# Two chained top-1 expert layers: the second layer's router scores taken from the first layer's output matmuls

## Chip, cores and metric

One Trainium2 chip, one core of it. Times are microseconds (us) of device time for one launch; lower is better. The engines are TensorE (PE: matmuls, and PEld: its weight loads), VectorE (DVE), ScalarE (ACT), GpSimd (POOL) and SyncE (SP); SP, ACT and POOL also issue DMAs, each in the order of its own program.

## What is computed

The reference has three stages over 14,336 tokens of 192 features: a causal 7-tap convolution along the sequence, a layer of experts with a skip rule and a residual, and a second layer of experts. Cut to what matters:

```python
x = conv(x, softmax(weight))                     # 4 x 3584 tokens, D = 192
# layer 1 (m = 0): E = 8 experts, F = 1024
do_compute = x @ w_skip > 0
e = argmax(x @ w_gate);  gate = softmax(x @ w_gate)[e]
x1 = x + (gate * (relu(x @ w1[e]) @ w2[e]) if do_compute else 0)
# layer 2 (m = 1): its own experts, a second gate
e = argmax(x1 @ w_gate2); gate = softmax(x1 @ w_gate2)[e]
out = gate * sigmoid(x1 @ w_output_gate2)[e] * (relu(x1 @ w1'[e]) @ w2'[e])
```

## The kernel before

All five engines run programs written out by hand; order on an engine is program order, and semaphores alone order the engines among each other. There is no scheduler.

**The front** (`Fori(0, B)` by `GPB` = 4, so 16 groups of 896 tokens) convolves, transposes the rows, computes the 25 router scores of each token (`scoreT`: skip, gate 1, gate 2, output gate 2), picks the bucket of each token, and scatters the rows of 196 floats into DRAM with 7 indirect DMAs per group from POOL (L432). Tokens that layer 1 computes go to buckets 0 to 7, skipped ones directly to a bucket of layer 2 (8 to 15).

**The expert stages** (`m` = 0, then 1) walk tiles of 256 tokens, expert by expert: 33 tiles for m = 0, 60 for m = 1. A tile g on PE: the hidden matmuls of four pairs c (L1086, L1095), then for each of 8 chunks j the output matmuls into banks 4 and 6 (L1110 with the high part `hh`, 384 columns, since high and low half of `w2` lie side by side; L1117 with the low part `hl`, 192 columns). ACT turns each pair into `hh` (L607), DVE into `hl` (L815, `h_low`). The rows of the tile with their gate come by a DMA that ACT issues between pairs 1 and 2 into the one buffer `xkeep` (L612). DVE's `result` multiplies the banks by the gate and adds x (L885, L891).

**Routing inside m = 0.** The rows that tile g-1 produced are routed to layer 2 while tile g is computed. PE transposes `y_rows` (L1045, L1046), ACT copies the transposes out (L565, L566), PE multiplies them with the second layer's gates (L1056, L1057, fp32). On DVE `choose` finds the expert (L831 to L845), `gate` its weight (L851 to L857), and `places` the row in the bucket (L864 to L872), for which PE counts ranks (L1063, L1065) after chunk j = 5. POOL's `send` does this in order: wait until the DMAs of the previous send have landed (`sent`), copy `y_rows` into `s_rows` (L447) and signal `copied`, take a quarter of the next expert's `w2` (L419), wait for `slots` from `places`, and issue two indirect DMAs (L453). In DVE's program of tile g the order is: `h_low` 0, `flags`, `h_low` 1 and 2, a piece of the next expert's w1 (L686), `h_low` 3, `x_turn` (L802, L803), `choose`, `x_low` (L808, L809), `gate`, `places`, `result`.

The waits that matter, before:

```python
# POOL, send(r)
pool.wait_ge(s["sent"], r * 32 + 16)
nc.gpsimd.tensor_copy(s_rows[:], y_rows[:]).then_inc(s["copied"], 1)
# ACT, tile g, between pairs 1 and 2
act.wait_ge(s["yrows_ready"], g + 1)
act.dma_start(xkeep[:], tile_rows(g, off)).then_inc(s["keep_in"], 16)
```

Of the kernel before, what the change touches and what calls it, by code (L numbers as in the profile page):

```python
# [24 lines left out]
FAR = 1.0e6  # L25
# [5 lines left out]
def program(nc, x, weight_rev, w_skip, gate1, gate2, out_gate2, w1_all, w2_all, out):  # L31
# [5 lines left out]
    HD = D // H  # L37
# [13 lines left out]
    ROW = D + 4  # L51
    GATE, TOK = D, D + 1
# [13 lines left out]
    with ctx:  # L66
# [3 lines left out]
        def sem(name):  # L70
# [11 lines left out]
        routerB = sb("routerB", [128, QUAD])  # L82
        rank_down = sb("rank_down", [128, E])
# [11 lines left out]
        xwin = sb("xwin", [W, GPB, WPG, D])  # L95
# [4 lines left out]
        scoreT = sb("scoreT", [128, 2, W])  # L100
        tok_int = sb("tok_int", [128, GPB * WPG], I32)
# [37 lines left out]
        w2 = sb("w2", [128, 2, FC, 2, D], F32R)  # L139
# [7 lines left out]
        y_part = sb("y_part", [128, SUB, D])  # L147
        s_rows = sb("s_rows", [128, SUB, ROW])
        yT = sb("yT", [128, 2, T])
        out_i = sb("out_i", [128, SUB], I32)  # L150

        SC = bank[7][:, 0:2 * W].rearrange("p (h i) -> p h i", i=W)

# [3 lines left out]
        consts_in, consts_pool, kern_in, kern_step, kern_out, toep_in, kern_e = map(sem, (  # L157
            "consts_in", "consts_pool", "kern_in", "kern_step", "kern_out", "toep_in", "kern_e"))
# [3 lines left out]
        win_in = [sem(f"win_in{q}") for q in range(GPB)]  # L162
# [3 lines left out]
            "scoreT_ready", "scoreT_copied", "scores_ready", "z_ready", "e_ready", "hot_ready", "rank_ready"))  # L166
        slots_ready, route_step, ones_ready, counted, table_step, tables_ready, first_filled, filled = map(sem, (
# [7 lines left out]
                 "y_ready", "yrows_ready", "yT_ready", "yT_copied", "scores", "z",  # L175
# [51 lines left out]

        def load_weights(eng, expert, par, f=slice(0, F), c=slice(0, FC), count=16 * PIECES):
# [41 lines left out]

        def settle(eng):


            eng.sem_inc(settled, 1)
# [7 lines left out]
        def _(sp):  # L282
            sp.dma_start(kern[:], weight_rev).then_inc(kern_in, 16)

            def load_windows(b, q):

                at = (b * S + q * WPG * W) * D
                sp.dma_start(xwin[:, q, :, :], bass.AP(windows.tensor, at, [[D, W], [W * D, WPG], [1, D]])
                             ).then_inc(win_in[q], 16)
                first = 1 if q == 0 else 0  # L290
                for k in range(4):
                    sp.dma_start(xhalo[k * QUAD:k * QUAD + HALO, q, first:, :],
                                 bass.AP(windows.tensor, at + (first * W - HALO) * D + k * HD2,
                                         [[D, HALO], [W * D, WPG - first], [1, HD2]])).then_inc(win_in[q], 16)
# [5 lines left out]
            sp.dma_start(toep[:], bass.AP(rev_w.tensor, 0, [[1, W], [TAPS_PAD, H], [1, W]])  # L300
                         ).then_inc(toep_in, 16)

            for q in range(1, GPB):
                load_windows(0, q)
# [91 lines left out]
        def _(pool):  # L396
# [39 lines left out]
            for m in range(2):  # L436
# [27 lines left out]
                with pool.Fori(0, E // 2) as half:  # L464
                    for par in range(2):
                        e = half * 2 + par
                        first, end = tiles.of(e)
                        def piece(i):
                            low2(e + (m * E + 1), 1 - par, i)
# [687 lines left out]
```

## Time and profile before

| | |
|---|---|
| median of 3 runs | 1124.97 us (1124.86 to 1124.97) |
| the profiled execution | 1125.92 us, span 1124.0 us |
| PE busy | 1052.6 us, 94% |
| DVE busy | 705.7 us, 63% |
| ACT busy | 528.2 us, 47% |
| POOL busy | 383.2 us, 34% |
| chain that ended last | PE 83%, issue 6%, POOL 4% |

The span is what the trace covers; the 1.9 us beyond it lie outside. Busy shares are means over three stages with different limits, so the argument goes by stage: the front ends near 183 us with POOL's last scatter, m = 0 runs from there to about 558 us, m = 1 to the end. A busy share of PE counts overlapping matmuls, so distances between starts are used for what a matmul costs.

### The profile page before, as it was taken

How to read it: one execution, taken by the hardware profiler on the slowest of the kernel's cores; microseconds unless marked ns; L12 is line 12 of the kernel's file. 1: busy time of each engine (PE TensorE's matmuls, PEld its weight loads, DVE VectorE, ACT ScalarE, POOL GpSimd, SP SyncE). 2: the span in 40 equal slices, each digit the busy share in tenths (PEclk: the TensorE clock that was granted, in tenths of full speed). 3: DMA queues.
4: the chain of work that ended last, by engine and by line, in shares of the span. 5: the costliest groups of instructions: out<-in, count | busy, mean ns of one | idle time of the engine just before them, and what ended most of it. 6: DMA issues, size and time to landing. Idle time of an engine off the chain costs nothing.

```text
span 1124.0 us, 32029 instructions
## 1 busy us (share of the span) xinstructions
PE 1052.6 (94%) x8478; PEld 991.9 (88%) x8479; DVE 705.7 (63%) x2264; ACT 528.2 (47%) x1190; POOL 383.2 (34%) x420
## 2 busy tenths in 40 slices
PE   6888756999999999999699999999999999999997
PEld 6666645999999999999699999999999999999997
DVE  0555663787888888888745565555555556565554
ACT  1545531444444444545345455554545455454443
POOL 2577774233323333333313232222323223223212
PEclk8998986999999999999889999999999999999999
DMA  8654424433434344434253343433434334223332
GB/s 235 196 155 155 129 83 138 116 87 84 87 80 96 85 99 100 90 82 107 58 141 95 74 110 66 111 81 80 114 78 114 64 93 96 63 59 69 63 64 49
DMA packets 252850, 110.90 MB, mean 99 GB/s; under 512 B 170499, under 2 KB 247798, under 8 KB 252832
## 3 DMA queue, kind: packets, MB, share of 16 engines
q1 hardware_dynamic: 210856, 62.45, 26.3%
q0 software_dynamic: 14560, 27.96, 7.1%
q10 hardware_dynamic: 27416, 20.30, 6.6%
q14 instruction: 13, 0.11, 0.0%
q8 instruction: 5, 0.08, 0.0%
HBM read 79.48 MB, written 33.08 MB: 100 GB/s over the span
## 4 chain that ended last, share of the span: by engine, by line
PE 83%; issue 6%; POOL 4%; DVE 2%; DMA 2%; ACT 1%; ACTq 1%; POOLq 0%; SPq 0%; DVEq 0%
PE bank L1095 32%; PE bank L1110 26%; PE bank L1117 12%; PE bank L1086 5%; POOL buckets L432 4%; PE bank L1057 2%; PE bank L1056 1%; PE bank L955 1%; DMA buckets<-rows,slot_i 1%; PE bank L1045 1%; PE bank L1046 1%; ACT rows L519 1%; PE bank L1018 1%; PE bank L1019 0%; DMA toep_halo<-rev_w 0%
## 5 line engine op out<-in xcount | busy, mean ns | idle before, releaser
L1110 PE MATMUL bank<-w,hh 128*128 128x384 f32 x1488 | 444.3, 361 | 1.0 <-DVE hl L815 1.0
L1117 PE MATMUL bank<-w,hl 128*128 128x192 f32 x1488 | 363.8, 255 | 0.0
L815 DVE SCALAR_TENSOR_TENSOR hl<-bank,hh 128x512 fp32r<-128x512 f32 x372 | 252.6, 689 | 127.4 <-ACT hh L607 124.5
L607 ACT ACTIVATE hh<-bank 128x512 fp32r<-128x512 f32 x372 | 221.4, 598 | 161.5 <-PE bank L1095 155.5
L1117 PEld LDWEIGHTS bank<-w,hl 128*128 128x128 f32 x1488 | 282.8, 191 | 0.0
L1110 PEld LDWEIGHTS bank<-w,hh 128*128 128x128 f32 x1488 | 280.2, 188 | 2.1 <-DVE hl L815 1.2
L458 POOL DMA_INDIRECT out<-y_rows,out_i x120 | 117.3, 978 | 413.9 <-DVE out_i L893 382.6
L1095 PE MATMUL bank<-xAh,w1h 128*128 128x256 f32 x744 | 222.5, 299 | 0.0
L1095 PE MATMUL bank<-xAh,w1l 128*128 128x256 f32 x744 | 209.9, 282 | 0.0
L1095 PE MATMUL bank<-xB,w1h 128*128 128x256 f32 x744 | 208.7, 281 | 0.0
L1095 PE MATMUL bank<-xAl,w1h 128*128 128x256 f32 x744 | 208.1, 280 | 0.0
L1095 PEld LDWEIGHTS bank<-xAh,w1h 128*128 128x128 f32 x744 | 141.8, 191 | 12.8 <-issue 0.7
L1095 PEld LDWEIGHTS bank<-xAh,w1l 128*128 128x128 f32 x744 | 141.8, 191 | 0.0
L1095 PEld LDWEIGHTS bank<-xAl,w1h 128*128 128x128 f32 x744 | 141.3, 190 | 0.0
L1095 PEld LDWEIGHTS bank<-xB,w1h 128*128 128x128 f32 x744 | 140.7, 189 | 0.0
L432 POOL DMA_INDIRECT buckets<-rows,slot_i x112 | 111.7, 997 | 63.3 <-issue 32.9
L453 POOL DMA_INDIRECT buckets<-s_rows,slot_i x68 | 66.9, 984 | 174.9 <-DVE slot_i L872 151.6
L559 ACT CAST xAh<-xT 128x256 fp32r<-128x256 f32 x95 | 38.6, 407 | 162.1 <-DVE xT L803 162.1
L891 DVE SCALAR_TENSOR_TENSOR y_rows<-bank,xkeep,y_part 128x192 f32<-128x192 f32 x186 | 68.6, 411 | 33.3 <-ACT y_part L578 33.3
L808 DVE TENSOR_TENSOR xAl<-xT,xAh 128x256 fp32r<-128x256 f32 x95 | 40.4, 425 | 75.0 <-ACT xC L561 75.0
L578 ACT ACTIVATE y_part<-bank,xkeep 128x192 f32<-128x192 f32 x120 | 43.9, 417 | 88.3 <-PE bank L1110 88.3
L1086 PE MATMUL bank<-xB,w1l 64*128 64x256 f32 x372 | 69.7, 307 | 13.9 <-DVE xB L809 13.9
(157 smaller groups left out, 1377.5 us busy)
## 6 DMA issues: line engine op xcount, KB each, us to landing
xblocks<-buckets SPq DMA_DIRECT2D x570, 32.0 KB, 1.8
xkeep<-buckets ACTq DMA_DIRECT2D x93, 196.0 KB, 2.7
xwin<-x SPq DMA_DIRECT2D x17, 672.0 KB
raw<-w_all SPq DMA_DIRECT2D x56, 192.0 KB
raw<-w_all SPq DMA_DIRECT2D x56, 128.0 KB
raw<-w_all SPq DMA_DIRECT2D x112, 64.0 KB
out<-y_rows,out_i POOLq DMA_INDIRECT x120
buckets<-rows,slot_i POOLq DMA_INDIRECT x112
```

The source lines that it names most:

```text
L432: nc.gpsimd.indirect_dma_start(out=buckets, out_offset=bass.IndirectOffsetOnAxis(ap=slot_i[0:W, q % 2, t:t + 1], axis=0), in_=rows[0:W, q, ...
L453: nc.gpsimd.indirect_dma_start(out=buckets, out_offset=bass.IndirectOffsetOnAxis(ap=slot_i[:, 0, h:h + 1], axis=0), in_=s_rows[:, h, :], i ...
L458: nc.gpsimd.indirect_dma_start(out=out, out_offset=bass.IndirectOffsetOnAxis(ap=out_i[:, h:h + 1], axis=0), in_=y_rows[:, h, 0:D], in_offs ...
L578: nc.scalar.mul(y_part[:, h, :], bank[Y[h]][:, 0:D], xkeep[:, h, GATE:GATE + 1]).then_inc(s["y_part"], 1)
L607: nc.scalar.activation(hh[:, 2 * c:2 * c + 2, :].rearrange("p c t -> p (c t)"), bank[c][:], ACT.Relu).then_inc(s["h_high"], 1)
L808: nc.vector.tensor_tensor(xAl[:], xT[:, 0, :], xAh[:].bitcast(F32), ALU.subtract)
L815: nc.vector.scalar_tensor_tensor(hl[:, 2 * c:2 * c + 2, :].rearrange("p c t -> p (c t)"), bank[c][:], 0.0, h, ALU.max, ALU.subtract).then_ ...
L891: nc.vector.scalar_tensor_tensor(y_rows[:, h, 0:D], bank[Y[h]][:, D:2 * D], gated, y_part[:, h, :], ALU.mult, ALU.add)
L1086: nc.tensor.matmul(bank[c + rows_at][:, u * T:(u + 1) * T], w1l[k0, par, 1, at * 128:(at + 1) * 128], (xB, xC)[rows_at][k0, :], start=(u = ...
L1095: last = nc.tensor.matmul(o, w[:, par, half_, f], xs[:], start=False, stop=(i == 3), skip_group_check=True)
L1110: return nc.tensor.matmul(bank[Y[h]][:, 0:2 * D], hh[:, j, t], w2[:, par, j, :, :].rearrange("p a d -> p (a d)"), start=(j == 0), stop=(j ...
L1117: last = nc.tensor.matmul(bank[Y[h]][:, 0:D], hl[:, j, t], w2[:, par, j, 0, :], start=False, stop=False)
```

## The change

In m = 0 the second layer's scores no longer come from the transposed result. The score of a row is (x + gate * h w2) G, and that is xG + gate * h (w2 G). So the front multiplies G (16 columns: `w_gate2` and the negated output gate) into every expert's `w2` once (`fold`), for which it loads `w2` of the 8 experts in halves, one half per group, transposes it, copies it, multiplies it with the router and transposes the result back. The output matmuls of m = 0 get 16 more columns per half (DS = 208 for 192), and every row carries xG: rows have 212 floats.

In the tile loop of m = 0 this removes the transposes, the copies `yT` and the fp32 score matmuls. x is no longer added by DVE in `result`: ACT's `y_half` now also runs for m = 0 (two multiplications by the gate), DVE does the second half only, and POOL's `send` adds `xkeep` to `y_rows` where it copied, so that it reads `xkeep`. `choose` reads the scores from `s_rows` and waits for `copied`; the load of the next `xkeep` waits for `copied` as well. `flags` moves behind `places`. At the start the Toeplitz matrix is loaded in two halves by two queues, the first convolution waits for the first half alone, and `xwin` has two buffers where it had four.

```diff
@@ POOL, send(r), m == 0
                         pool.wait_ge(s["sent"], r * 32 + 16)
                         settle(pool)
-                        nc.gpsimd.tensor_copy(s_rows[:], y_rows[:]).then_inc(s["copied"], 1)
+                        nc.gpsimd.tensor_tensor(s_rows[:, :, 0:DS], y_rows[:, :, 0:DS], xkeep[:, :, 0:DS], ALU.add)
+                        nc.gpsimd.tensor_copy(s_rows[:, :, TOK], xkeep[:, :, TOK]).then_inc(s["copied"], 1)
                         between()
                         pool.wait_ge(s["slots"], r + 2)
@@ ACT, tile g
                                 if c == 1:
-                                    act.wait_ge(s["yrows_ready"], g + 1)
+                                    act.wait_ge(s["copied" if m == 0 else "yrows_ready"], g + 1)
                                     act.dma_start(xkeep[:], tile_rows(g, off)
                                                   ).then_inc(s["keep_in"], 16)
-                                    if m == 0:
-                                        yT_copy(g)
                             x_high(g + 1)
                             if m == 0:
                                 exp(g)
-                            if m == 1:
-                                y_half(g)
+                            y_half(g)
@@ DVE
                 def choose(step, r):
-                    dve.wait_ge(s["scores"], r + 1)
+                    dve.wait_ge(s["copied"], r + 1)
...
                     if m == 0:
                         dve.wait_ge(s["copied"], g + 1)
-                        dve.wait_ge(s["yT_ready"], g + 1)
                     else:
                         dve.wait_ge(s["sent"], g * 32 + 16)
-                    for h in range(SUB):
-                        gated = xkeep[:, h, GATE:GATE + 1]
-                        if m == 0:
-                            nc.vector.scalar_tensor_tensor(y_part[:, h, :], bank[Y[h]][:, 0:D], gated,
-                                                           xkeep[:, h, 0:D], ALU.mult, ALU.add
-                                                           ).then_inc(s["y_part"], 1)
+                        nc.vector.tensor_copy(out_i[:], xkeep[:, :, TOK])
@@ PE, tile g
-                                if m == 0 and c == 1:
-                                    transpose_y(g)
-                            if m == 0:
-                                scores(g)
                             pe.wait_ge(s["yrows_ready"], g + 1)
...
                                         return nc.tensor.matmul(
-                                            bank[Y[h]][:, 0:2 * D], hh[:, j, t],
-                                            w2[:, par, j, :, :].rearrange("p a d -> p (a d)"),
+                                            bank[Y[h]][:, 0:2 * DS].rearrange("p (a d) -> p a d", d=DS)[:, :, 0:width],
+                                            hh[:, j, t], w2[:, par, j, :, 0:width],
                                             start=(j == 0), stop=(j == FC - 1))
@@ PE, front, end of a group
-                    pe.wait_ge(tr_copied, n * 2 + 3)
+                    pe.wait_ge(tr_copied, n * 3 + 3)
+                    pe.wait_ge(w2raw_in[q % 2], b * 64 + (q // 2 * 32 + 32))
+                    for i in range(HC):
+                        nc.tensor.transpose(bank[4][:, i * W:(i + 1) * W], w2_rawA[:, q % 2, i, :], ident[:])
+                    for i in range(2):
+                        last = nc.tensor.transpose(bank[5][:, i * W:(i + 1) * W],
...
+                    pe.wait_ge(tr_copied, n * 3 + 4)
+                    for k in range(4):
+                        nc.tensor.matmul(SCW[k * QUAD:(k + 1) * QUAD, :], routerA[:], w2tA[:, k * W:(k + 1) * W],
+                                         start=False, stop=False, skip_group_check=True)
@@ ACT, front, a group
                     rows_out(n + 1, (q + 1) % GPB)
+                    act.wait_ge(tr_ready, n * 3 + 3)
+                    nc.scalar.copy(w2tA[:], bank[4][:])
+                    nc.scalar.copy(w2tB[:], bank[5][:, 0:2 * W]).then_inc(tr_copied, 1)
@@ DVE, front, ahead of the scores' sum
+                    nc.vector.tensor_copy(rows[0:W, q, :, D:DS], LG[:, :, 1 + E:NR])
```

What this does to the order on two engines. On ACT, inside a tile of m = 0, before the change (`hh` is the high part of the hidden layer, `yT` the copied transposes):

```order
L607 ACTIVATE hh<-bank 128x512 [waits m0_h_ready]
L612 ISA [waits m0_yrows_ready]
L612 DMA xkeep<-buckets 128x2x196
L565 COPY yT<-bank 128x256 [waits m0_yT_ready]
L566 COPY yT<-bank 64x256
L606 REGISTER_ALU
L607 ACTIVATE hh<-bank 128x512 [waits m0_h_ready]
```

and after it, from the same place to the end of the tile:

```order
L653 ACTIVATE hh<-bank 128x512 [waits m0_h_ready]
L658 ISA [waits m0_copied]
L658 DMA xkeep<-buckets 128x2x212
L652 REGISTER_ALU
L653 ACTIVATE hh<-bank 128x512 [waits m0_h_ready]
...
L609 CAST xAh<-xT 128x256 [waits m0_x_trans]
L610 CAST xB<-xT 64x256
L611 CAST xC<-xT 64x256
L615 ACTIVATE escore<-score 128x2x9 [waits m0_z]
L620 ISA
L623 ACTIVATE y_part<-bank,xkeep 128x208 [waits m0_y_ready,m0_keep_in]
```

The two copies are gone, two multiplications stand at the end, and what stands ahead of the third `hh` now waits for a signal of POOL where it waited for one of DVE.

On POOL, one `send` of m = 0, before the change:

```order
L445 ISA [waits m0_yrows_ready]
L447 COPY s_rows<-y_rows 128x392 [waits m0_sent]
...
L419 ISA [waits w_high]
...
L419 TENSOR_TENSOR w<-raw,w 128x2x192
...
L453 DMA buckets<-s_rows,slot_i 233472x196 [waits m0_slots]
```

and after it:

```order
L490 ISA [waits m0_yrows_ready]
L492 TENSOR_TENSOR s_rows<-y_rows,xkeep 128x2x208 [waits m0_sent]
L493 COPY s_rows<-xkeep 128x2
...
L462 TENSOR_TENSOR w<-fold,w 128x2x16
L464 ISA x2
L464 TENSOR_TENSOR w<-raw,w 128x2x192
...
L499 DMA buckets<-s_rows,slot_i 233472x212 [waits m0_slots]
```

The signal `copied` comes from L447 before and from L493 after; both stand behind the wait for `sent`. The order of the DMAs is as it was.

## Rows read from the trace of the kernel before

**Rows 1.** Windows by stage: length, busy us of PE, PEld, DVE, ACT, POOL, PEclk, DMA

```profile
129.60:133.00 3.40, 1.98 (x12) 1.94 (x13) 0.33 (x3) 3.04 (x10) 2.78 (x3) 0.80 0.26 89
205.00:549.00 344.00, 344.00 (x2698) 327.83 (x2698) 280.37 (x1049) 164.22 (x366) 110.61 (x121) 1.00 0.39 90
```

**Rows 2.** Chain that ended last: start us, us, what; tiles of m = 0, then m = 1

```profile
217.98 2.08 PE bank L1095 x16
...
229.08 2.07 PE bank L1095 x16
...
585.64 3.94 PE bank L1095 x32
594.83 3.94 PE bank L1095 x32
```

**Rows 3.** Timeline of PE in a tile of m = 0, end of the output matmuls

```profile
438.06 0.36 PE L1110 MATMUL bank<-w,hh 128*128 128x384 f32 x1
438.26 0.25 PE L1117 MATMUL bank<-w,hl 128*128 128x192 f32 x1
438.35 0.36 PE L1110 MATMUL bank<-w,hh 128*128 128x384 f32 x1
```

**Rows 4.** Timeline of POOL, the send beside that tile

```profile
430.24 0.98 POOL L453 DMA_INDIRECT buckets<-s_rows,slot_i  x1 [0.30 <-DVE y_rows L893]
433.59 1.03 POOL L447 COPY s_rows<-y_rows 128x392 f32<-128x392 f32 x1 [2.37 <-DMA buckets<-s_rows,slot_i]
...
440.05 0.99 POOL L453 DMA_INDIRECT buckets<-s_rows,slot_i  x1 [4.44 <-DVE slot_i L872]
```

**Rows 5.** Groups of POOL: count, busy us, mean ns, idle before and its releaser

```profile
L419 POOL TENSOR_TENSOR w<-raw,w x56 | 59.4, 1061 | 1.5
...
L447 POOL COPY s_rows<-y_rows 128x392 f32<-128x392 f32 x34 | 21.2, 623 | 84.6 <-DMA buckets<-s_rows,slot_i 84.6
```

**Rows 6.** Timeline of ACT in the same tile

```profile
431.18 0.39 ACTq L612 DMA_DIRECT2D xkeep<-buckets  x1
431.61 0.37 ACT L565 COPY yT<-bank 128x256 f32<-128x256 f32 x1
...
432.34 0.60 ACT L607 ACTIVATE hh<-bank 128x512 fp32r<-128x512 f32 x1
```

**Rows 7.** Timeline of DVE in the same tile

```profile
432.97 0.69 DVE L815 SCALAR_TENSOR_TENSOR hl<-bank,hh 128x512 fp32r<-128x512 f32 x1 [0.65 <-ACT hh L607]
433.57 0.68 DVE L686 TENSOR_TENSOR w1l<-raw,w1h  x1
434.17 0.68 DVE L815 SCALAR_TENSOR_TENSOR hl<-bank,hh 128x512 fp32r<-128x512 f32 x1
...
435.46 0.13 DVE L831 TENSOR_REDUCE top<-bank 128x2 f32<-128x16 f32 x1
...
436.77 0.43 DVE L808 TENSOR_TENSOR xAl<-xT,xAh 128x256 fp32r<-128x256 f32 x1
...
439.00 0.16 DVE L872 TENSOR_TENSOR slot_i<-slot,flag 128x2 int32<-128x2 f32 x1
```

**Rows 8.** All of L872: count, min/median/max ns, first and last start us

```profile
L872 DVE TENSOR_TENSOR slot_i<-slot,flag x34: 160/161/165, 193.5 to 558.3; 128x2 int32<-128x2 f32 x34
```

**Rows 9.** All of the front's scatters: count, ns, first and last start us

```profile
L432 POOL DMA_INDIRECT buckets<-rows,slot_i x112: 978/980/1482, 37.4 to 181.9; - x112
```

**Rows 10.** Waits of PE: the first convolution's, us, times, longest

```profile
PE bank L955 <- DMA toep_halo<-rev_w: 5.1, 1, 5.1
```

**Rows 11.** Timeline of a group in the front, PE and ACT

```profile
60.56 0.32 PE L1018 MATMUL bank<-ident,rows 128*128 128x128 f32 x1 [0.67 <-ACT rows L519]
...
61.69 0.59 ACT L537 COPY x1A<-bank 128x512 f32<-128x512 f32 x1 [0.94 <-PE bank L1019]
...
66.64 0.63 PE L1028 MATMUL bank<-x1A,routerA 128*32 128x256 f32 x8
...
68.37 0.32 PE L1018 MATMUL bank<-ident,rows 128*128 128x128 f32 x1 [0.67 <-ACT rows L519]
```

More of the change, by code:

```diff
@@ L890, in result @@
                         dve.wait_ge(s["y_part"], g * SUB + (h + 1))
[L891 to L894 removed]
+                        last = nc.vector.scalar_tensor_tensor(y_rows[:, h, 0:width], bank[Y[h]][:, DS:DS + width],
+                                                              gated, y_part[:, h, 0:width], ALU.mult, ALU.add)
+                    last.then_inc(s["yrows_ready"], 1)
+                width = DS if m == 0 else D
                 if m == 0:
@@ L916, in _ @@
                             step = Steps(s["step"], g * STEPS2)
-                            h_low(g, 0)
-                            if m == 0:
-                                flags(step, g)
-                            for c in range(1, PAIRS):
+                            for c in range(PAIRS):
                                 h_low(g, c)
@@ L930, in _ @@
                                 places(step, g)
+                                flags(step, g)
                                 assert step.n == STEPS2
@@ L939, in _ @@
                     step = Steps(s["step"], n * STEPS2)
-                    for part in (flags, choose, gate, places):
+                    for part in (choose, gate, places):
                         part(step, n)
@@ new lines, in _ @@
+                    last.then_inc(tr_ready, 1)
+                    pe.wait_ge(scoreT_copied, n + 1)
+                    pe.wait_ge(setup_done, 8)
+                    pe.wait_ge(fold_ready, n)
+                    for k in range(4):
+                        used = 1 if k == 3 else 2
+                        nc.tensor.matmul(SC[k * QUAD:(k + 1) * QUAD, 0:used, :], routerA[:],
+                                         x1A[:, 0:used, k * W:(k + 1) * W], start=True, stop=False,
+                                         skip_group_check=True)
@@ new lines, in _ @@
+                    for k in range(4):
+                        used = 1 if k == 3 else 2
+                        nc.tensor.matmul(SC[k * QUAD:(k + 1) * QUAD, 0:used, :], routerB[:],
+                                         x1B[:, 0:used, k * W:(k + 1) * W], start=False, stop=False,
+                                         skip_group_check=True)
+                    pe.wait_ge(tr_copied, n * 3 + 4)
+                    for k in range(4):
+                        nc.tensor.matmul(SCW[k * QUAD:(k + 1) * QUAD, :], routerA[:], w2tA[:, k * W:(k + 1) * W],
+                                         start=False, stop=False, skip_group_check=True)
@@ L1031, in _ @@
+                    for k in range(4):
+                        last = nc.tensor.matmul(SCW[k * QUAD:(k + 1) * QUAD, :], (routerB, routerC)[k % 2][:],
+                                                w2tB[:, k // 2 * W:(k // 2 + 1) * W], start=False, stop=True,
+                                                skip_group_check=True)
                     last.then_inc(scoreT_ready, 1)
```

213 lines of the change are left out of this document (114 added, 99 removed).

## Prediction

> **What bounds the kernel now.** I read the windows by stage first. From 205 to 549 us, the tiles of m = 0, PE is busy all 344 us at its full clock and nothing else is: DVE 280, ACT 164, POOL 111 [rows 1]. The chain that ended last says the same: the same matmuls come back every 11.10 us in m = 0 and every 9.19 us in m = 1 [rows 2]. So in m = 0 PE's own work sets the pace, and whatever leaves PE is worth its time until another chain is longer. That chain is what I looked for next, in the timelines of POOL, ACT and DVE beside one tile. The front is different: POOL starts its 112 scatters at 37.4 us and the last at 181.9 [rows 9], 1.29 us each (0.98 and a gap of 0.30), 9.0 us per group, while PE, where nothing holds it, goes round in 7.81 us (60.56 to 68.37) [rows 11]. There POOL is the bound.
>
> **What PE gets back in m = 0.** A tile of m = 0 differs from one of m = 1 by 11.10 - 9.19 = 1.91 us: transposes, score matmuls and rank matmuls [rows 2]. The ranks stay, so 1.91 is the most that can go. Added are 32 columns to each of 16 matmuls with 384 and 16 columns to each of 16 with 192. Start to start these take 0.20 and 0.09 us [rows 3]; in proportion 16 x 0.017 + 16 x 0.008 = 0.39 us. Net 1.5 us a tile, and 33 tiles (34 sends with the last one [rows 8]) make 50 us, if PE stays the bound.
>
> **What the new wait closes.** It does not stay the bound, I think. Before, ACT loaded `xkeep` and went on to pair 2 as soon as DVE's `result` was done. Now it waits for `copied`, and POOL raises that only after the two DMAs of the previous send have landed. The row of L447 shows that this landing is late already: POOL sat idle ahead of the copy for 84.6 us, 2.56 per send, always for the landing [rows 5]. Before, only `gate` on DVE needed that signal, 4 us later. Now what is behind the waiting instruction on ACT is the load and `hh` of pairs 2 and 3; DVE's `h_low` 2 and 3 wait for these; behind them in DVE's order are `x_turn`, `choose`, `x_low`, `gate` and `places`; and `places` gives the slots for which POOL's next DMAs wait. That is a loop of one tile. Its length, from `copied` on:
>
> 1. ACT: the load's issue takes 0.43 us until the next instruction starts (431.18 to 431.61) [rows 6], and for the signal and the register operations ahead of it I add 0.15, an estimate; I take 0.6 to the start of the third `hh`.
> 2. From the start of the third `hh` (432.34) to the end of `slot_i` (439.16): 6.82 us [rows 6, 7]. It holds one `hh` (0.60), two `h_low` and a piece of w1 at 0.60 each, `x_turn`, `choose` (435.46 to 436.77), `x_low`, `gate`, `places`. None of this changes: DVE works through it back to back, the row after `h_low` 2 shows no idle [rows 7]. The fourth `hh` ends before its turn on DVE comes. I count nothing for `choose` reading SBUF where it read PSUM.
> 3. POOL: from the end of `slot_i` to the DMA 0.89 us (439.16 to 440.05) [rows 4, 7], two DMAs 0.98 + 0.30 + 0.98 = 2.26, then the landing. The tile shows 2.37 [rows 4], the mean is 2.56 [rows 5]; I take the mean. The rows grow by 8%, the packets not in number.
> 4. POOL: the addition. No row has it. Nearest is L419, two inputs, 384 elements, 1.06 us [rows 5]: 416 elements make 1.15, and the small copy of the token numbers 0.1. The lower end is the one-input copy of 392 elements in the tile without disturbance, some 0.6 (its mean is 0.62 [rows 5]). I take 1.25.
>
> Sum: 0.6 + 6.82 + 0.89 + 2.26 + 2.56 + 1.25 = 14.4 us. The w1 piece (0.60) is in four tiles of each of seven experts, 28 of 33, so the mean is 14.3. The GPSIMD Engine Reference of the Trainium skill, section 3.1, puts a two-input operation at about 2.6 cycles an element, bound by the shared read port. By that, at 1.2 GHz, 416 elements would be an estimated 0.90 us and not 1.15, and the whole forecast 8 us lower; the row decides.
>
> So a tile takes 14.3 where it took 11.1. Neither end is inside PE: with 9.6 us of work it has about 4.7 us to wait, first for `hl` of pair 2, then for `z` ahead of the ranks. ACT's two new multiplications, DVE's shorter `result` and the moved `flags` (three short operations behind `slot_i`) lie beside POOL's DMAs and cost nothing; without that cover they would cost 1 us. The fold's extra pieces (16 columns on ACT and POOL) lie behind `copied`, where POOL waits for slots anyway.
>
> Summed from the first `slot_i` to the last, 364.8 us before (193.5 to 558.3) [rows 8]: now 32 rounds of 14.3, and one short one that ends with `choose` to `places` alone (435.46 to 439.16 less 0.89 for `x_low` = 2.8) behind 0.89 + 2.26 + 2.56 + 1.25 = 7.0. That is 457.6 + 9.8 = 467.4, so +102.6 us.
>
> **The front.** PE's round gets longer: the six transposes of `w2` and the router's matmuls lie beside ACT's copy of the rows, but then ACT copies 128x512 and 128x256 out (0.59 for the first [rows 11], about 0.9 together), PE does eight more router matmuls (0.63 for as many [rows 11]), and the scores' sum on DVE waits for one more copy (0.2). Less what overlaps, 7.81 becomes 9.2 to 9.7, against POOL's 9.0; I take 9.4, so PE with ACT becomes the bound: 15 rounds x 0.4 = +6. Ahead of it the first convolution waited 5.1 us for the halo DMA behind the whole matrix [rows 10]; half the matrix, and one DVE operation for seven, give back an estimated 3.5, of which a longer first round takes 1.4 back off again for the first slot. Net +3 to +4; I take +3. Ends: -3 if the round stays below 9.0, +8 at 9.7. m = 1 is bound by PE and unchanged; `out_i` only moves ahead within `result`.
>
> **Sum**, against the profiled execution's span: 1124.0 + 102.6 + 3 = 1229.6. The median of the runs (1124.97) lies 1 us above that span, so 1230.6; I forecast 1230.
>
> **Rivals.**
> - *The loop is hidden, PE stays the bound: faster.* Place: the wait for `copied` on ACT. It would be hidden if the loop were under 9.6 us, so 4.7 less than I add up; from 11.1 on the change costs. For it: ACT and DVE are far from full [rows 1]. Against: terms that are nearly all measured, and POOL's idle in every send [rows 5]. It would give 1125 - 50 + 3 = 1078. 8%.
> - *No change*: the loop comes out between, near 11.1, for instance with a landing that the lighter DMA load makes much faster. 1120 to 1130, the middle is 1125. 3%.
> - *PE falls to its low clock and becomes part of the loop.* In the front a stretch with PE busy 1.98 of 3.40 us shows a granted clock of 0.80 [rows 1], so part of it at 1.2 GHz, not 2.4. With 4.7 idle of 14.3 us this can happen in every tile. It changes nothing as long as the slower part adds less than those 4.7 us; at 1.2 GHz for the whole tile PE needs near 18 us, and 33 x 3.7 = +122 over my sum, 1350; half of that is likelier. The Trainium skill's TensorE: Matmul & The Clock Gate, Part 1 (HAM oscillation), says that idle gaps between bursts of matmuls bring the half clock back each time round; by it the clock would dip in every tile of m = 0, and this rival be near. But a PE at half clock also fills its idle time, which ends the reason for the dip. 5%.
>
> **How the numbers follow.** The slow loop as added up 84%, hidden 8%, no change 3%, low clock 5%. Own range of the likeliest: the loop from 13.4 (addition 0.6, landing 2.37) to 15.3 (1.0 more, as far up as down, for a landing or an addition that is slower than its row) is 32 x 0.9 to 1.0 = 29 to 32 either way, with the front's ends 1192 to 1268. That holds most of 84% and the near part of the low clock, about 8 in 10. Measurement tells 0.2% apart, 2.2 us. Faster by more 9%, within 2%, slower 89%.
>
> **What would show it.** Right: starts of L653 for pair 2 right behind L493 and the load; the period of m = 0 at 14 to 14.6 us; POOL idle some 2.5 us ahead of L492 and about 7 ahead of L499's slots; PE busy near 70% in m = 0, waiting for `hl` and for `z`; last `slot_i` near 660 us. The addition L492 at 1.1 to 1.2 us. In the front, rounds of 9.2 to 9.7 us. Wrong: a period under 11 with PE busy throughout, or PE's clock below 0.8 in m = 0.

## Result and the profile after

The changed kernel takes 1239.61 us (median of 4 runs, 1238.14 to 1241.54) against 1124.97: ratio 1.1014, 95% interval [1.0995, 1.1032]. The forecast was 1230, slower. The profiled execution took 1239.93 us, its span 1237.9. Some runs of some kernels are slower for no reason of the kernel's (one of e5 took 1547.95 us, one of e7 3313.76): the medians here and below count them, the ratios do not, so a ratio need not be the quotient of two medians.

The page of the changed kernel: busy time, share and instructions of each engine, and the chain that ended last.

```profile
PE 1089.8 (88%) x8438; PEld 1001.7 (81%) x8439; DVE 685.6 (55%) x2197; ACT 546.1 (44%) x1272; POOL 406.5 (33%) x487
...
PE 52%; DVE 12%; issue 12%; DMA 9%; POOL 4%; ACT 3%; POOLq 2%; ACTq 2%; DVEq 1%; SPq 1%
```

PE had 83% of that chain before; now DVE, DMA and issue share a third of it. The same windows as in [rows 1], one inside m = 0 and one inside m = 1:

```profile
215.00:660.00 445.00, 363.52 (x2336) 328.14 (x2336) 255.69 (x967) 165.84 (x396) 131.18 (x180) 0.86 0.32 72
690.00:1230.00 540.00, 540.00 (x4216) 521.54 (x4215) 312.31 (x673) 273.07 (x582) 144.41 (x146) 1.00 0.37 85
```

In m = 0 PE is busy 82% of the time at a granted clock of 0.86, where it was 100% at 1.00; m = 1 is as before. Two lists of all instructions on a line, which answer to [rows 8] and to L447 in [rows 5] (count, min/median/max ns, first and last start); under the second, what POOL waited for ahead of the addition:

```profile
L919 DVE TENSOR_TENSOR slot_i<-slot,flag x34: 160/160/163, 202.4 to 669.9; 128x2 int32<-128x2 f32 x34
...
L492 POOL TENSOR_TENSOR s_rows<-y_rows,xkeep x34: 1053/1078/1117, 190.0 to 665.7; 128x416 f32<-128x416 f32 x34
...
  DMA buckets<-s_rows,slot_i: 78.8, 33
```

From the first `slot_i` to the last it is 467.5 us, 364.8 before [rows 8]. So of the 113.9 us that the span grew by, 102.7 are in the tiles of m = 0, 8.9 ahead of them (first `slot_i` at 202.4, not 193.5) and the other 2.3 behind them.

The waits by pairs of lines (total us, times, longest):

```profile
POOL buckets L499 <- DVE slot_i L919: 239.4, 33, 7.9
...
ACT hh L653 <- POOL s_rows L493: 97.2, 29, 5.8
...
PE bank L1108 <- DVE score L893: 60.0, 34, 8.1
...
PE bank L1158 <- DVE hl L862: 35.3, 23, 3.5
```

And one turn of the loop, in the timelines of POOL, ACT and DVE:

```profile
450.95 1.07 POOL L492 TENSOR_TENSOR s_rows<-y_rows,xkeep 128x416 f32<-128x416 f32 x1 [2.58 <-DMA buckets<-s_rows,slot_i]
451.98 0.18 POOL L493 COPY s_rows<-xkeep 128x2 f32<-128x2 f32 x1
...
460.60 0.99 POOL L499 DMA_INDIRECT buckets<-s_rows,slot_i  x1 [7.26 <-DVE slot_i L919]
461.89 0.99 POOL L499 DMA_INDIRECT buckets<-s_rows,slot_i  x1 [0.30 <-issue]
...
452.39 0.38 ACTq L658 DMA_DIRECT2D xkeep<-buckets  x1
452.89 1.08 ACT L653 ACTIVATE hh<-bank 128x512 fp32r<-128x512 f32 x2 [2.75 <-POOL s_rows L493]
...
453.52 0.69 DVE L862 SCALAR_TENSOR_TENSOR hl<-bank,hh 128x512 fp32r<-128x512 f32 x1 [2.66 <-ACT hh L653]
...
459.55 0.16 DVE L919 TENSOR_TENSOR slot_i<-slot,flag 128x2 int32<-128x2 f32 x1
```

Read it as a circle. POOL waits 2.58 us for the landing, adds and copies for 1.21 (450.95 to 452.16). ACT gets `copied` and starts the third `hh` 0.73 later (452.89). From there to the end of `slot_i` (459.71) it is 6.82, 0.89 more to POOL's DMA, 2.28 for both DMAs, and a landing again, 2.39 in the mean (78.8 by 33). Together 1.21 + 0.73 + 6.82 + 0.89 + 2.28 + 2.39 = 14.3 us. The distances from one `slot_i` to the next have the mean 14.32 over the first 32 rounds, single ones lie between 12.95 and 15.25.

### The profile page after: what moved, and what is told of

It reads as the page before. It is cut to its first block, busy times and chain, and to the rows that moved or that the text cites. A ratio compares the mean times of both kernels' runs of the same rounds, so it can differ in the third digit from the quotient of the medians.

```text
span 1237.9 us, 32239 instructions
## 1 busy us (share of the span) xinstructions
PE 1089.8 (88%) x8438; PEld 1001.7 (81%) x8439; DVE 685.6 (55%) x2197; ACT 546.1 (44%) x1272; POOL 406.5 (33%) x487
## 4 chain that ended last, share of the span: by engine, by line
PE 52%; DVE 12%; issue 12%; DMA 9%; POOL 4%; ACT 3%; POOLq 2%; ACTq 2%; DVEq 1%; SPq 1%
PE bank L1140 19%; PE bank L1151 17%; DMA buckets<-s_rows,slot_i 8%; PE bank L1158 8%; PE bank L1131 3%; POOL buckets L477 3%; DVE hl L862 2%; ACT hh L653 2%; ACTq L658 1%; PE bank L996 1%; DVE xT L849 1%; DVE xT L850 1%; ACT rows L566 1%; DVE xB L856 1%; DVE y_rows L932 1%
## 5 line engine op out<-in xcount | busy, mean ns | idle before, releaser
L1151 PE MATMUL bank<-w,hh 128*128 128x384 f32 (+1 forms) x1488 | 476.2, 377 | 1.1 <-DVE hl L862 0.9
L1158 PE MATMUL bank<-w,hl 128*128 128x192 f32 (+1 forms) x1488 | 382.1, 267 | 35.5 <-DVE hl L862 35.3
L1158 PEld LDWEIGHTS bank<-w,hl 128*128 128x128 f32 x1488 | 293.9, 198 | 42.9 <-DVE hl L862 42.5
L1151 PEld LDWEIGHTS bank<-w,hh 128*128 128x128 f32 x1488 | 293.5, 197 | 4.2 <-DVE hl L862 2.1
L504 POOL DMA_INDIRECT out<-y_rows,out_i x120 | 117.3, 978 | 416.3 <-DVE y_rows L932 385.1
L1140 PE MATMUL bank<-xAl,w1h 128*128 128x256 f32 x744 | 214.2, 288 | 0.0
L1140 PEld LDWEIGHTS bank<-xAl,w1h 128*128 128x128 f32 x744 | 146.9, 197 | 0.0
L1140 PEld LDWEIGHTS bank<-xB,w1h 128*128 128x128 f32 x744 | 145.0, 195 | 0.0
L623 ACT ACTIVATE y_part<-bank,xkeep 128x192 f32<-128x192 f32 (+1 forms) x186 | 69.1, 422 | 161.2 <-PE bank L1151 161.2
L1131 PE MATMUL bank<-xB,w1l 64*128 64x256 f32 x372 | 80.8, 345 | 14.5 <-DVE xB L856 13.4
L1131 PEld LDWEIGHTS bank<-xB,w1l 64*128 64x128 f32 x372 | 59.5, 222 | 35.9 <-issue 22.2
```

The source lines that it names most:

```text
L504: nc.gpsimd.indirect_dma_start(out=out, out_offset=bass.IndirectOffsetOnAxis(ap=out_i[:, h:h + 1], axis=0), in_=y_rows[:, h, 0:D], in_offs ...
L623: nc.scalar.mul(y_part[:, h, 0:width], bank[Y[h]][:, 0:width], xkeep[:, h, GATE:GATE + 1]).then_inc(s["y_part"], 1)
L1131: nc.tensor.matmul(bank[c + rows_at][:, u * T:(u + 1) * T], w1l[k0, par, 1, at * 128:(at + 1) * 128], (xB, xC)[rows_at][k0, :], start=(u = ...
L1140: last = nc.tensor.matmul(o, w[:, par, half_, f], xs[:], start=False, stop=(i == 3), skip_group_check=True)
L1151: return nc.tensor.matmul(bank[Y[h]][:, 0:2 * DS].rearrange("p (a d) -> p a d", d=DS)[:, :, 0:width], hh[:, j, t], w2[:, par, j, :, 0:widt ...
L1158: last = nc.tensor.matmul(bank[Y[h]][:, 0:width], hl[:, j, t], w2[:, par, j, 0, 0:width], start=False, stop=False)
```

## Experiments

Totals can't be set side by side across all of them. On two of the chips (e1 to e4, e9 to e11) the front ran some 80 to 100 us longer in every profiled kernel, m = 1 some 5 to 8 us longer, and the kernel before took 1212.76 and 1201.36 us there. So the table gives the distance from the first `slot_i` to the last, which lies behind the front, and each ratio is to the kernel before on the same chip. On those two chips even the ratio carries the front: e9's stage is 15 us shorter than the 364.8 of the kernel before, its ratio is above 1. That the stage itself compares across chips rests on the changed kernel's: 467.5, 465.8 (e8) and 466.6 (e11, which leaves m = 0 as it is).

| run | edit | first to last `slot_i` | median | kernel before there | ratio [95%] |
|---|---|---|---|---|---|
| e1 | load behind the 4th `hh` | 381.3 | 1251.68 | 1212.76 | 1.043 [1.030, 1.056] |
| e2 | addition in its own buffer | 391.8 | 1263.35 | 1212.76 | 1.049 [1.038, 1.060] |
| e3 | both | 369.5 | 1244.66 | 1212.76 | 1.032 [1.022, 1.042] |
| e4 | addition twice | 494.9 | 1377.99 | 1212.76 | 1.145 [1.134, 1.156] |
| e5 | kernel before with the wait alone | 491.0 | 1251.04 | 1125.34 | 1.110 [1.108, 1.112] |
| e6 | e3, ranks behind the last chunk | 365.3 | 1137.20 | 1125.34 | 1.009 [1.007, 1.011] |
| e7 | e6, `w2` halves first in the front | 363.7 | 1129.34 | 1125.34 | 1.004 [1.002, 1.006] |
| e8 | the changed kernel again | 465.8 | 1236.09 | 1125.34 | 1.099 [1.096, 1.102] |
| e9 | e7, w1 piece ahead of `result` | 350.1 | 1210.92 | 1201.36 | 1.008 [1.004, 1.013] |
| e10 | e9, ranks back behind chunk 5 | 353.7 | 1215.18 | 1201.36 | 1.017 [1.011, 1.022] |
| e11 | changed kernel, no gap in the columns | 466.6 | 1332.13 | 1201.36 | 1.113 [1.107, 1.120] |
| e12 | e7, w1 piece behind `x_low` | 329.7 | 1098.03 | 1125.24 | 0.977 [0.975, 0.979] |

### Is it the loop, and is it the wait?

**e1.** The load of the next `xkeep` moves behind the fourth `hh`, so that nothing of the hidden layer is queued behind the wait.

```diff
-                                if c == 1:
+                                if c == (3 if m == 0 else 1):
                                     act.wait_ge(s["copied" if m == 0 else "yrows_ready"], g + 1)
```

> The changed kernel with one edit: in m = 0 ACT waits for `copied` and loads `xkeep` behind the fourth `hh` and not between the second and the third. Loop theory: third and fourth `hh` and the four `h_low` leave the loop, it runs from `copied` straight into `choose`: 3.7 us on DVE, 0.9 to the DMA, 2.3 for two DMAs, 2.4 landing, 1.3 addition, 0.2 of signals, so about 10.9 us a tile for 14.3. 33 tiles: about -108, near 1132 us (1125 to 1142). Rival A (DVE's order itself is the bound, ACT's wait only lies beside it): above 1200. Rival B (PE at its low clock is part of the loop): the clock in m = 0 stays near 0.86 and the time above 1160.

The stage shrinks from 467.5 to 381.3, so the two `hh` behind the wait were in the loop. The tile is 11.6 in the mean (372.1 by 32 rounds), over the 10.9 expected, and the stage falls by 86 and not by 108. One thing that the sum left out shows in the trace: in about half of the tiles the small copy L493, whose end signals `copied`, takes 0.65 us or more and not the usual 0.18. At 502.03 us, for one, a piece of w1 runs on DVE beside it; e7 below tells why that matters. Whether that makes all of the 0.7 stays open.

**e2.** POOL adds into a buffer of its own, `y_mid`, without waiting for the landing, signals `copied`, and copies to `s_rows` after the landing. `choose` reads `y_mid`.

```diff
-                        pool.wait_ge(s["sent"], r * 32 + 16)
-                        nc.gpsimd.tensor_tensor(s_rows[:, :, 0:DS], ...)
+                        nc.gpsimd.tensor_tensor(y_mid[:, :, 0:DS], ...)
                         ...
                         between()
+                        pool.wait_ge(s["sent"], r * 32 + 16)
+                        nc.gpsimd.tensor_copy(s_rows[:], y_mid[:]).then_inc(s["moved"], 1)
```

> The changed kernel with one edit: POOL adds into a buffer of its own (`y_mid`), raises `copied` there without waiting for the landing, and copies into `s_rows` after the landing; `choose` reads `y_mid`, and DVE waits for that second copy only ahead of writing the gate. ACT's load stays between second and third `hh`. Loop theory: the landing (2.4 us) leaves the loop, all else stays: 11.9 us a tile, 33 x -2.4 = -79, near 1161 us (1150 to 1172). Rival A (the landing is not in the loop, since POOL waits anyway): 1239, no change. Rival B (the second copy, about 0.6, comes into the loop): near 1180.

Most tiles take 11.96 to 12.0 us: 14.3 less the landing's 2.4, as expected. The landing is a term of the loop at its full size.

**e3.** Both edits.

> Both edits of the two kernels before. Loop theory: the loop falls to 8.5 us, below PE's own work, so PE is the bound: the 9.23 us of a tile of m = 1, the ranks (0.17) and the wider matmuls (0.39 at most), 9.8 us a tile, 33 x -4.4 = -145, near 1094 us (1087 to 1102), PE busy throughout in m = 0 at full clock. Rival (DVE or ACT becomes the bound at about 10.5 to 11): 1120 to 1135.

11.05 us where 9.8 was expected. A miss: PE waits for `z` ahead of the ranks (1.28 us in one tile, for L897 of this kernel), and something holds most tiles at 11.05. What that is came out with e6, e7 and e9.

**e4.** The addition a second time, into a spare buffer, ahead of the real one.

> The changed kernel; POOL does its addition twice, first into a buffer that nobody reads. Loop theory: every microsecond between landing and `copied` is paid in full: 33 to 34 x 1.08 = +36, near 1275 us (1270 to 1281). Rival A (another chain is as long, or PE is the bound): +0 to +10. Rival B (the clock of PE falls further and is part of the loop): more than +50.

+27.4 us over 467.5, not +36. The extra operation takes 1.09 us in the mean, and POOL's idle for the landing falls from 2.39 to 2.17 (71.6 by 33). So 33 x (1.09 - 0.22) = 29, near the 27.4: POOL's elementwise time goes into the loop, less what it gives back at the landing. Why the landing comes sooner was not tried.

**e5.** The kernel before with the one wait of ACT changed, and nothing else of the change.

```diff
-                                    act.wait_ge(s["yrows_ready"], g + 1)
+                                    act.wait_ge(s["copied" if m == 0 else "yrows_ready"], g + 1)
```

> The kernel before, with one part of the change alone: in m = 0 ACT's load of `xkeep` waits for `copied` and not for DVE's result. All transposes, score matmuls and the cheap copy stay. Loop theory: the same loop closes, with the copy (0.5) for the addition (1.25) and the two `yT` copies (0.65) on it, so about 14.2 us a tile for 11.1: from the first slot_i to the last +100 us, the total +100 (93 to 108) over the kernel before. Rival (the new work of the change, the addition on POOL or the wider matmuls, makes the loss): +0 to +20.

Ratio 1.110: the wait alone costs as much as the whole change and more, +126 us in the stage where 93 to 108 were expected. The timelines of one tile of it:

```profile
442.01 0.40 ACTq L612 DMA_DIRECT2D xkeep<-buckets  x1
442.45 0.37 ACT L565 COPY yT<-bank 128x256 f32<-128x256 f32 x1 [2.33 <-POOL s_rows L447]
442.72 0.36 ACT L566 COPY yT<-bank 64x256 f32<-64x256 f32 x1
442.99 1.08 ACT L607 ACTIVATE hh<-bank 128x512 fp32r<-128x512 f32 x2
...
443.14 0.40 PE L1056 MATMUL bank<-routerA,yT 128*128 128x16 f32 x2 [1.34 <-ACT yT L566]
...
446.12 0.58 PE L1110 MATMUL bank<-w,hh 128*128 128x384 f32 x1
...
446.65 0.57 PE L1110 MATMUL bank<-w,hh 128*128 128x384 f32 x1
...
449.55 0.19 PE L1063 MATMUL bank<-hot_pad,before 128*128 128x24 bf16 x1
...
449.83 0.17 DVE L864 TENSOR_TENSOR place<-bank,next_row 128x16 f32<-128x16 f32 x1 [0.88 <-PE bank L1065]
```

The copies `yT` stand between the load and the third `hh` (0.54); the expectation had them. It did not have the other: DVE waits for the ranks of PE, 0.88 here and 1.55 in the mean. From 220 to 670 us of this run:

```profile
DVE place L864 <- PE bank L1065: 46.4, 30, 2.4
```

So in this kernel the loop that closes goes through PE: `yT`, score matmuls, six chunks of output matmuls, ranks, `places`. And PE is slow there. Behind its wait of 1.34 us for `yT` the granted clock falls to 0.59 (445 to 447 us) and 0.65 (447 to 449.5), and the matmuls of L1110 start 0.53 us apart where they start 0.29 apart in the kernel before [rows 3]. From the first score matmul to the ranks it is 6.41 us; in the tile of the kernel before it is 4.72:

```profile
433.08 0.29 PE L1056 MATMUL bank<-routerA,yT 128*128 128x16 f32 x2
...
437.80 0.19 PE L1063 MATMUL bank<-hot_pad,before 128*128 128x24 bf16 x1
```

The 1.69 us between the two are more than the 0.88 that DVE waits. In sum, against the changed kernel's 14.32 a tile: +0.54 for `yT`, +1.55 for the ranks, -0.70 since POOL's copy takes 0.51 where addition and small copy take 1.21, -0.63 since the landing holds POOL up for 1.76 (58.2 by 33) and not 2.39: 15.08, and the stage less its short last round, 491.0 - 8.4, makes 15.08 by 32. So the experiment shows that the wait alone makes a loss of this size, but not that it makes it by the chain of the prediction alone: 1.55 of its 15.08 us are a wait for PE, which in the tile shown its low clock makes.

**e8.** The changed kernel again, on the chip of e5 to e7.

> The changed kernel as it is, on the chip of the three others, to compare stages on one chip. From the first slot_i to the last 467 us, as in its first profile (462 to 472); ratio to the kernel before 1.10 if this chip's front is undisturbed.

465.8: the stage repeats within 0.4%.

### What holds the tile at 11.05?

**e6.** e3 with the ranks behind chunk 7, so that PE need not wait for `z`.

```diff
-                                if m == 0 and j == 5:
+                                if m == 0 and j == 7:
```

> The kernel with the middle buffer and the late load, and PE's rank matmuls moved from behind chunk 5 to behind chunk 7. That kernel ran m = 0 at 11.05 us a tile with PE waiting for `z` ahead of the ranks, 1.3 us a tile. Theory: a second loop of one tile bounds it: z, ranks, chunks 6 and 7, the hidden matmuls of the next tile, `hh`, `h_low`, w1 piece, `x_turn`, `choose`. With the ranks last PE never waits for `z`: 9.8 us a tile, first slot_i to last near 323 us for 369.5 (320 to 332). Rival (DVE or ACT is the bound at about 11): no change, 365 to 370.

The stage is 365.3, not the 320 to 332 expected, so the wait for `z` is not what holds the tile. Most tiles stay at 11.05, and two of those without a piece of w1 take 9.1. That points to the piece itself.

**e7.** e6, and in the front SP issues the `w2` halves of a batch ahead of the two experts' weights.

```diff
+            def weights_after(q):
+                if q in (1, 3):
+                    load_weights(sp, q // 2, q // 2)
+            next_batch(1, weights_after)
```

> The kernel with middle buffer, late load and ranks last, and in the front SP issues the halves of w2 of the second batch ahead of the weights of experts 0 and 1 (those behind the second and fourth group of that batch). Theory: the one stall of PE in the front for a half of w2 (5.5 us) goes: the first slots of the third group come about 6.7 us after the usual round instead of behind a round of 16; total 5 to 8 us less than the kernel without this edit, and about 1090 us on a chip where the kernel before takes 1125 (ratio 0.97). Rival (the stall moves to windows or weights): less than 2 us.

The first `slot_i` comes at 194.3 us, not 202.4, as expected; the tiles stay at 11.05, so the total misses (ratio 1.004, expected 0.97). The timelines of POOL and DVE in one tile of e7 show the cause:

```profile
450.66 0.99 POOL L509 DMA_INDIRECT buckets<-s_rows,slot_i  x1 [5.29 <-DVE slot_i L930]
...
452.95 1.09 POOL L497 TENSOR_TENSOR y_mid<-y_rows,xkeep 128x416 f32<-128x416 f32 x1
...
454.35 1.02 POOL L471 TENSOR_TENSOR w<-raw,w  x1
455.31 0.99 POOL L504 COPY s_rows<-y_mid 128x424 f32<-128x424 f32 x1
...
453.36 2.55 DVE L737 TENSOR_TENSOR w1l<-raw,w1h  x1
455.84 0.68 DVE L872 SCALAR_TENSOR_TENSOR hl<-bank,hh 128x512 fp32r<-128x512 f32 x1
```

The piece of w1 (L737, both inputs in SBUF) takes 2.55 us; its median is 0.693. It starts while POOL adds and ends only 0.54 after POOL's piece of `w2` has ended (455.37). Then POOL's copy L504, whose median is 0.538, takes 0.99, 0.45 longer. This is what the Trainium skill says in "SBUF — State Buffer", section "SBUF: two separate sides": VectorE's operations with two SBUF inputs and GpSimd's share a pair of ports as an exclusive lock, and the one that comes second waits. The trace agrees, and shows that four operations of POOL in a row are waited out together. (The kernel before shows it too, [rows 4, 7]: POOL's copy at 433.59 takes 1.03 us beside the piece at 433.57; in e5 that copy takes 0.51.) It also makes the 11.05 a loop: DMA at 450.66, POOL's operations to 455.37, the rest of the piece to 455.84, `h_low` to `slot_i` at 460.81 (it starts at 460.65), and 0.89 to the next DMA, 461.70: 11.04. The same loop holds e3. There the piece starts later and takes 0.68 to 1.40 us, but in 17 of the 28 tiles that have a piece it ends 0.54 to 0.56 us behind POOL's piece of `w2`, as here; in five it ends 1.02 to 1.04 behind, and these tiles take about 11.55.

**e9.** The piece goes where POOL has no such operation, between `flags` and `result`.

```diff
-                                if c == 2 and m == 0:
-                                    pieces.one()
...
                                 flags(step, g)
...
-                            else:
-                                pieces.one()
+                            pieces.one()
                             result(g)
```

> This is the kernel of e7 (addition in a buffer of its own, xkeep load behind the fourth hh, ranks behind the last chunk, w2 halves ahead of the weights) with one more edit: DVE's piece of the next expert's w1 stands behind flags and ahead of result, where POOL has no tensor operation, and no longer behind the third h_low, where POOL adds. Theory: in e6 and e7 that piece takes 2.6 to 2.8 us instead of 0.68 because both of its inputs lie in SBUF and POOL works there at the same time; with it moved, the tiles of m = 0 come down from 11.05 to PE's 9.6 to 9.9 us, first slot_i to last 320 to 332 us, total 1085 to 1100 us, ratio 0.97. Rival: the piece was late for another reason (its own wait for w1h) and PE is bound at 11: then the period stays 11 and the total at 1129. Second rival: the piece only moves the stall, to result's multiplication or to x_low, with a period of 10.5 or so, total 1112.

Most tiles come down to 9.3 to 10.4 us, so the cause is right. Yet the stage misses the 320 to 332 expected: the last tile of four of the experts now takes 15, which no theory had, since PE needs the last piece for the next expert.

```profile
506.06 0.76 DVE L737 TENSOR_TENSOR w1l<-raw,w1h  x1 [0.35 <-issue]
...
507.19 0.57 PE L1139 MATMUL bank<-xB,w1l 64*128 64x256 f32 x1 [3.32 <-DVE w1l L737]
```

**e10.** e9 with the ranks back behind chunk 5.

> The kernel of e9 with the rank matmuls back behind chunk 5. It tells whether their place matters once the piece is out of the way. By the theory places and flags come 1 us earlier for POOL but PE has to wait for z behind chunk 5: DVE reaches z sooner by the piece's 0.7 to 2.8 us, so PE's wait of 1.3 us in e3 is gone, period again 9.6 to 9.9, total the same as e9 within 5 us. Rival: PE still waits for z, 0.5 to 1.3 us a tile, total 15 to 40 us over e9.

353.7 against 350.1, ordinary tiles some 10.1 for 9.7, the four long ones 13.8 to 13.9 for 15: their place is worth some 0.4 us in an ordinary tile once the piece is out of the way.

**e12.** The piece behind `x_low`: after POOL's operations and ahead of the expert's end. Its call behind `h_low` 2 goes, as in e9.

```diff
                             x_low(g + 1)
                             if m == 0:
+                                pieces.one()
                                 gate(step, g)
```

> The kernel of e9 with DVE's piece of w1 put between x_low and gate: behind POOL's addition and its piece of w2 (in e9 these end at 526.9 us and x_low at 528.7 us of the same tile), but about 3 us ahead of result, so that the last piece of an expert is there when TensorE begins the next expert. In e9 ordinary tiles took 9.3 to 10.2 us and each last tile of an expert 15 us, because TensorE waited up to 3.3 us for w1l and then had its bursts late. Theory: ordinary tiles 9.5 to 10.1 us, the tiles at an expert's end 9.8 to 11 us, first slot_i to last 320 to 335 us (350 in e9, 364 in e7, 365 in the kernel before); the total, if the chip's front is the usual one, 1088 to 1103 us, ratio 0.97 to 0.98. Rival: the tiles at an expert's end keep their 15 us because they wait for ACT's w1h or for the load of the raw weights, stage 350, ratio 0.99. Second rival: the piece delays z and places, DVE becomes the bound at 10.5 a tile, stage 345.

1098.03 us, ratio 0.9768 [0.975, 0.9786]: faster than both kernels, and the stage of 329.7 lies in the 320 to 335 expected. All pieces, and all `slot_i`:

```profile
L737 DVE TENSOR_TENSOR w1l<-raw,w1h x64: 680/692/693, 102.8 to 985.2; - x56, 128x512 fp32r<-128x512 f32 x8
...
L930 DVE TENSOR_TENSOR slot_i<-slot,flag x34: 160/160/164, 193.4 to 523.1; 128x2 int32<-128x2 f32 x34
```

A window inside its m = 0 (columns as in [rows 1]):

```profile
205.00:520.00 315.00, 296.20 (x2319) 285.58 (x2317) 271.42 (x966) 168.00 (x395) 151.11 (x215) 0.99 0.45 103
```

No piece takes over 0.70 any more, most tiles take 9.7 to 10.2 us, and PE is at 94% with its clock at 0.99. The stage, 329.7, is 35.1 shorter than before the change; the span, 1091.3, is 32.7 shorter.

### Where do m = 1's 2.3 us come from?

From the last `slot_i` to the end it is 565.7 us before and 568.0 after. The chain shows the tile:

```profile
688.06 3.95 PE bank L1140 x32
697.29 3.95 PE bank L1140 x32
```

9.23 us where [rows 2] has 9.19. **e11** lays the 2 x 192 columns side by side, in the bank and in what is read of `w2`, instead of 192 in each 208. It takes other columns of `w2` for that, so its output leaves out a part of the second layer's product; the work has the same size. DVE's `result` reads the bank accordingly (not shown).

```diff
-                                            bank[Y[h]][:, 0:2 * DS].rearrange("p (a d) -> p a d", d=DS)[:, :, 0:width],
-                                            hh[:, j, t], w2[:, par, j, :, 0:width],
+                                            bank[Y[h]][:, 0:2 * width],
+                                            hh[:, j, t],
+                                            w2[:, par, j, :, :].rearrange("p a d -> p (a d)")[:, 0:2 * width],
```

> The changed kernel with one edit in the output matmuls: their 2 x width columns lie side by side in the bank and are read side by side from w2 (for m = 1 that takes other columns of w2 than its halves, so the output leaves out a part of the second layer's product; the work has the same size). Theory: the 2.3 us by which m = 1 takes longer in the changed kernel (tile 9.227 for 9.187 us) come from the gap of 16 columns in the rows that the matmuls read or write; without the gap 9.19 us again, total 2.3 us lower, ratio to before 1.099. Rival: the tile stays at 9.23, then it is not the gap. In m = 0 there is no gap in either, so its stage stays at 467 us.

Its chain:

```profile
1213.06 3.96 PE bank L1140 x32
1222.29 3.96 PE bank L1140 x32
```

Still 9.23. It is not the gap; the cause stays open.

## Why the prediction was right

**The loop.** The mechanism and its place were right, shown by what was undone and what was doubled: moving the load takes 86 us of it away (e1), the landing counts in it in full (e2), POOL's elementwise time for about three quarters, most of the rest comes back at the landing (e4), and a kernel without it and without the lock is faster than before (e12). The wait alone makes a loss of this size too (e5), though there the loop goes through PE. The terms as forecast and as read: ACT 0.6 and 0.73; third `hh` to `slot_i` 6.82 and 6.82; 0.89 and 0.89; two DMAs 2.26 and 2.28; landing 2.56 and 2.39; addition and copy 1.25 and 1.21. Sum 14.3, stage 467.5 against 467.4. Two small misses, of ACT and of the landing, cancel, and so do 32 rounds of 14.32 for 14.3 and a short last one of 9.3 for 9.8. That the stage agrees to 0.1 us is luck; that it agrees to some per cent is not.

**The addition.** Its own row has 1.078 us against the 1.15 scaled from L419, nearer than the 0.90 estimated from the Trainium skill's GPSIMD Engine Reference, section 3.1. Scaling by a row of the same engine and the same kind of operands was the better source. What the rate leaves out is a fixed part: the addition of 32 elements beside it (L462, 0.24 us) would be 0.07 by that rate, which leaves 0.17, and 0.90 + 0.17 = 1.07 is an estimate near the row.

**The low clock.** The prediction had PE busy near 70% and named a clock below 0.8 as a sign of being wrong; it is 82% and 0.86. In the tile of the loop, PE's hidden matmuls start 0.21 us apart at first and 0.12 later:

```profile
460.85 0.41 PE L1140 MATMUL bank<-xAl,w1h 128*128 128x256 f32 x1
461.06 0.41 PE L1140 MATMUL bank<-xAh,w1l 128*128 128x256 f32 x1
...
461.88 0.28 PE L1140 MATMUL bank<-xAh,w1l 128*128 128x256 f32 x1
461.99 0.28 PE L1140 MATMUL bank<-xB,w1h 128*128 128x256 f32 x1
```

PE had waited 1.70 us ahead of the ranks of this tile before. So within a tile it falls to the lower of its two clocks, 1.2 GHz (granted clock 0.50 from 459.30 to 461.50 us), and comes back to 2.4, the third rival's mechanism. Here it is not in the loop, as that rival's bound said: PE fills part of its waiting with slower work. DVE never waits for the ranks in m = 0, and what the slow matmuls hold up is done before the loop asks for it: `y_rows` at 461.12 us, while POOL waits for the landing until 465.95. The trace agrees with the oscillation that the Trainium skill describes (TensorE: Matmul & The Clock Gate, Part 1), but here it lies inside slack. It need not: in e5 the slow part comes ahead of the ranks, and DVE waits for them 1.55 us a tile. The prediction gave this rival 5%; in e5, with the transposes and score matmuls still on PE, it comes true in part.

**The front: a term mis-sized.** "Net +3 to +4; I take +3", with +8 as its upper end; it measured +8.9. The rounds themselves came out near the forecast, nearly all between 9.1 and 9.5 us. One round takes 16.35, in which PE waits once for a `w2` half and POOL for the slots behind it:

```profile
PE bank L1068 <- DMA w_rawB<-w_all: 5.5, 1, 5.5
...
59.50 0.98 POOL L477 DMA_INDIRECT buckets<-rows,slot_i  x1 [7.27 <-DVE slot_i L805]
```

That half is issued by SP behind the weights of two experts. The prediction counted the fold's work and not the order of its DMAs on their queue. e7 moved them and got 8.2 us back at the first `slot_i` (202.5 in e6 to 194.3). Without the stall the front would have cost 0.8 us (194.3 for 193.5), less than the 3 of the sum, so that term was too high and the missing one larger than the miss shows.

**m = 1: a term of 2.3 us taken as nothing.** Its size is measured, its cause is not found.

Of the 8.3 us between the summed span (1229.6) and the measured one (1237.9), 5.9 are the front's, 2.3 those of m = 1 and 0.1 the loop's.

**The rival that PE stays the bound** priced the gain at 50 us with a loop under 9.6. e12 shows it is real, though smaller: 35 us in the stage, with most tiles at 9.7 to 10.2 us for 9.6.

## What to carry to other kernels

- A wait on an in-order queue costs what stands behind it, not what it guards. Before adding one, follow the signal back to its latest releaser and forward through everything queued behind; if the path closes on itself, its length is the new period, and slack in busy shares (here ACT 47%, DVE 63%) says nothing.
- Work moved to POOL has two prices: its own time, and that of DVE's operations with two SBUF inputs that it overlaps. Once the long loop is cut, place those operations of DVE where POOL has nothing elementwise, but ahead of their consumer's deadline. That alone made 34 us here (e7 to e12).
- A wait that leaves TensorE idle can also slow its next work. What that costs is told by what stands behind: nothing in the changed kernel, where the loop does not wait for the slow part, 1.55 us a tile in e5, where the ranks do stand behind it.
- A new DMA on a shared queue is priced by what is queued ahead of it.

## What the runs showed of the hardware

- The lock between DVE and POOL costs the latecomer the whole run of the other's operations: a piece of 0.69 us took up to 3.1 (its maximum in e7), and a copy of 0.54 took 0.999 when it was second.
- TensorE's granted clock fell to 0.50 to 0.59 in each of the 33 rounds of m = 0 in the changed kernel, and to 0.50 in 32 of the 33 of e5. In the tiles shown it fell behind a wait of 1.70 us ahead of the ranks in the changed kernel (0.50 for the 2.2 us from 459.30 us), and behind one of 1.34 us for `yT` in e5 (0.59 and 0.65 from 445 to 449.5 us). In the kernel before, which has no such wait, it is 1.00 from 205 to 549 us.
- One operation of DVE over 7 elements whose input is read backwards took longer than seven operations of one element each. After, and then before the change:

```profile
3.48 1.48 DVE L706 TENSOR_SCALAR kern_pad<-kern_exp,kern_sum 8x7 f32<-8x7 f32 x1
```

```profile
3.38 0.93 DVE L665 TENSOR_SCALAR kern_pad<-kern_exp,kern_sum 8x1 f32<-8x1 f32 x7
```

  1.48 us against 0.93. Whether the reading direction is the cause wasn't tried.
- The front took 80 to 100 us longer on two of the chips, while m = 0 did not change: e11, with the changed kernel's m = 0, has its first `slot_i` at 289.5 us and a stage of 466.6; e8 has 200.6 and 465.8. From the last `slot_i` to the end it was 573.3 for 568.1. Why was not tried.
